# Soft and top-1 mixture of experts behind an attention stage: waits moved in the expert loop, one transpose a tile, a table with long runs, a sort with unit strides

## What is computed

```python
# attention, for each of 8 batches and 8 heads (S=512, Ns=32, D=64)
xread = softmax(x @ state.T / 8) @ state ; sread = softmax(state @ x.T / 8) @ x
x = concat(xread, sread)                        # 4352 rows of 512
# soft mixture: 32 slots, 4 for each of 8 experts
logits = x @ phi ; d = softmax(logits, over rows) ; c = softmax(logits, over slots)
slot_out[e] = relu((d.T @ x)[e] @ w1[e]) @ w2[e]
x = c @ slot_out
# top-1 mixture: each row goes to one of 8 experts
e = argmax(x @ w_gate) ; gate = softmax(x @ w_gate)[e] * sigmoid(x @ w_output_gate)[e]
out = gate * (relu(x @ v1[e]) @ v2[e])
```

## Time and profile before

| | |
|---|---|
| median of 3 runs | 518.16 us (517.82 to 519.98) |
| the profiled execution | 520.96 us, span 519.2 us |
| PE busy | 454.6 us, 88% of the span |
| PEld | 241.8 us |
| DVE, ACT, POOL | 132.7, 127.7, 127.8 us |
| the chain that ended last | PE 66%, DMA 14%, ACT 5%, issue 5%, DVE 5% |
| in it | output matmuls (858) 48%, the table's transfer 5%, weight units 5% |
| DMA | 87.20 MB, 168 GB/s over the span |

### The profile page before, as it was taken

How to read it: one execution, slowest core, us unless ns; L and a number is a source line. 1 busy time by engine, 2 the same in 40 slices (tenths; PEclk the granted TensorE clock), 3 DMA queues, 4 the chain that set the end, 5 groups by cost and what they waited for, 6 DMA issues and landing times.

```text
span 519.2 us, 9941 instructions
## 1 busy us (share of the span) xinstructions
PE 454.6 (88%) x3705; PEld 241.8 (47%) x3706; DVE 132.7 (26%) x315; ACT 127.7 (25%) x329; POOL 127.8 (25%) x191
## 2 busy tenths in 40 slices
PE   7888786799898793999999999999999999999991
PEld 5676655663435462444444444444444444444440
DVE  2689698820004601101010101010101010101000
ACT  3978554300001101212121212121212121212110
POOL 2433513040021004032222222232323232323110
PEclk9999898789796966999999999999999999999997
DMA  8799546779999998678601010101010101010110
GB/s 284 251 348 296 212 164 203 286 281 391 432 425 428 427 394 283 232 231 294 232 22 43 22 43 22 43 22 43 22 43 21 43 22 42 26 39 24 38 44 3
DMA packets 29306, 87.20 MB, mean 168 GB/s; under 512 B 5942, under 2 KB 15704, under 8 KB 26200
## 3 DMA queue, kind: packets, MB, share of 16 engines
q1 hardware_dynamic: 24016, 76.65, 39.3%
q0 software_dynamic: 3952, 9.49, 5.4%
q10 hardware_dynamic: 1304, 0.57, 0.4%
HBM read 77.25 MB, written 9.75 MB: 168 GB/s over the span
## 4 chain that ended last, share of the span: by engine, by line
PE 66%; DMA 14%; ACT 5%; issue 5%; DVE 5%; SPq 2%; POOL 1%; ACTq 0%; POOLq 0%; DVEq 0%
PE bank L858 48%; DMA token_rows<-z 5%; DMA arena<-in_moe_w 5%; DMA arena<-in_x 3%; PE bank L846 3%; PE bank L741 2%; SPq L287 2%; ACT z L1015 2%; PE bank L529 1%; PE bank L835 1%; DMA z<-token_rows,sidx 1%; PE bank L789 1%; PE bank L518 1%; PE bank L570 1%; PE bank L592 1%
## 5 line engine op out<-in xcount | busy, mean ns | idle before, releaser
L858 PE MATMUL bank<-arena,z 128*128 x560 | 249.3, 598 | 15.6 <-ACT z L1015 10.1
L858 PEld LDWEIGHTS bank<-arena,z 128*128 128x128 f32 x560 | 103.6, 190 | 139.6 <-issue 139.6
L1313 DVE TENSOR_SCALAR z<-bank 128x256 f32<-128x256 f32 x70 | 26.4, 419 | 260.2 <-PE bank L846 260.2
L1022 ACT ACTIVATE z<-bank,tile_gate 128x512 f32<-128x512 f32 x35 | 24.0, 687 | 242.0 <-PE bank L858 242.0
L449 POOL COPY rows_to<-sidx 128x1 int32 (+1 forms) x35 | 6.3, 181 | 167.9 <-ACT z L1022 167.9
L468 POOL DMA_INDIRECT out<-z,rows_to x35 | 36.7, 1049 | 29.8 <-POOL rows_to L449 29.8
L453 POOL DMA_INDIRECT z<-token_rows,rows_from x32 | 33.6, 1050 | 25.6 <-POOL rows_from L449 25.6
L846 PE MATMUL bank<-cT,parts 32*128 32x128 f32 x560 | 26.0, 300 | 0.0
L1015 ACT ACTIVATE z<-bank 128x256 f32<-128x256 f32 x70 | 23.0, 381 | 3.1 <-PE bank L846 1.1
L835 PE MATMUL bank<-ident,z 128*32 128x128 f32 x280 | 15.4, 292 | 9.1 <-DMA z<-token_rows,sidx 9.1
L846 PEld LDWEIGHTS bank<-cT,parts 32*128 32x128 f32 x560 | 19.2, 189 | 7.7 <-issue 7.7
(11 more groups left out here) (205 smaller groups left out, 416.5 us busy)
## 6 DMA issues: line engine op xcount, KB each, us to landing
arena<-in_moe_w SPq DMA_DIRECT2D x29, 2048.0 KB, 12.1
arena<-in_x SPq DMA_DIRECT2D x7, 1024.0 KB, 8.8
parts<-in_moe_w SPq DMA_DIRECT2D x3, 2048.0 KB, 13.1
arena<-in_x SPq DMA_DIRECT2D x2, 512.0 KB, 5.7
out<-z,rows_to POOLq DMA_INDIRECT x35, 3.0
token_rows<-z ACTq DMA_DIRECT2D x1, 528.0 KB
z<-in_state SPq DMA_DIRECT2D x1, 512.0 KB, 3.6
z<-in_state SPq DMA_DIRECT2D x8, 64.0 KB, 8.2
```

What stands on the lines that cost most here:

```text
L858: mm = e.matmul(pY[p][:, :], hT[p][:, c, :], arena[:, bass.ds(ex * UNIT + 512 * c, 512)], start=(c == 0), stop=(c == CF - 1))
L1022: e.activation(ysb[p], pY[p][:, :], ACT.Copy, scale=tile_gate[:, q:q + 1])\
L1313: e.tensor_scalar(hT[p][:, 2 * g:2 * g + 2, :], bank[g][:, 0:GW].rearrange("p (c t) -> p c t", c=2), 0.0, None, ALU.max).then_inc(relu_v, 1)
```

## The change

In the loop, TensorE's load of the expert's number and all waits for output(t) stand at the head of the step, ahead of turn_c(t+2) and hidden(t+1); the waits of hidden for the relu go, and each relu signals once instead of twice. The turning is one 128x128 transpose of `c4`, four copies side by side of the gathered rows, which VectorE lays out (`turned_rows`) behind its wait for the row. The table has a row of 34 floats: combine weights, gate, and the row's number in the output; it is written in one transfer with one contiguous run for each partition, and it begins with 102 rows that name no output row (`no_row`, written early through SP's queue). The sort gives the row's place in the table, as the upper bits of a float32; places that stay empty lead to such a row. The scatter takes its row numbers from the gathered rows. `lane_mat`, `tile_hot` and `tile_id` go: for each of 34 tiles VectorE writes `lane_hot[:, t, :]` and `tile_row[:, t, :]` with a scalar operation each, and TensorE's sort waits tile by tile. `count_experts` stands after expert 0 instead of 1. The foldings' operands are written chunk by chunk, so that they are read with unit stride. Three groups of `keep_clock` (4, 4, 6) stand in front of waits after w2. The first eight units (`EARLY = 8`) are loaded in four transfers each, of 4 KB a partition instead of 16 KB.

```diff
         def w_loaded(u):
-            return 16 * sum(1 for v in range(u + 1) if SLOT[v] == SLOT[u])
+            return 16 * sum(pieces(v) for v in range(u + 1) if SLOT[v] == SLOT[u])
...
-                e.dma_start(slot(SLOT[u]).rearrange("p (c n) -> p c n", c=c),
-                            src[ex].rearrange("(p c) n -> p c n", p=P)).then_inc(w_in[SLOT[u]], 16)
+                rows = src[ex].rearrange("(p c) n -> p (c n)", p=P)
+                step = UNIT // pieces(u)
+                for a in range(0, UNIT, step):
+                    e.dma_start(slot(SLOT[u])[:, a:a + step], rows[:, a:a + step]).then_inc(w_in[SLOT[u]], 16)
             for b in range(1, 4):
                 load_x(b)
+            e.wait_ge(no_row_ready, 2)
+            e.dma_start(table[0:FIRST_ROW, :], no_row[:, :]).then_inc(table_out, 16)
...
+            e.tensor_copy(rowbuf[:, :, GATE_W + 1], rowid[:, :]).then_inc(row_ready, 1)
...
-            e.wait_ge(w_used, 2 * NE)
-            e.tensor_copy(lane_mat, lane[:, :].unsqueeze(2).to_broadcast([P, P, NT])).then_inc(lanes_laid, 1)
...
-                numbers(rows_to[:, q % 2:q % 2 + 1], t, to_copied, t + 1)
+                e.tensor_copy(rows_to[:, q % 2:q % 2 + 1], gate_to[:, q, 1:2]).then_inc(to_copied, 1)
...
-                mm = e.matmul(pF[:, NS * c:NS * c + NS], every(siP, c, CD), foldn[:, :], start=True, stop=True)
+                mm = e.matmul(pF[:, NS * c:NS * c + NS], siP[:, P * c:P * c + P], foldn[:, :], start=True, stop=True)
...
             def sort_rows():
-                e.wait_ge(lane_ready, 3)
                 for t in range(NT):
-                    mm = e.matmul(pT[:, 0:2 * ST], lane_hot[:, :, t], tile_id[:, :, :, t], start=(t == 0),
-                                  stop=(t == NT - 1))
+                    e.wait_ge(lane_ready, 2 * t + 2)
+                    mm = e.matmul(pT[:, 0:ST], lane_hot[:, t, :], tile_row[:, t, :], start=(t == 0), stop=(t == NT - 1))
...
-                if ex == 1:
+                if ex == 0:
                     count_experts()
...
-                e.wait_ge(row_in[q], 4 * (t - q) + 16)
-                for g in range(4):
-                    mm = e.matmul(pC[NS * g:NS * g + NS, :], row[q][:, 0:NS], ident[:, :], start=True, stop=True)
-                mm.then_inc(c_psum, 1)
+                e.wait_ge(c4_ready, t + 1)
+                e.transpose(pC, c4[q % 2], ident[:, :]).then_inc(c_psum, 1)
...
-                if wait:
-                    e.wait_ge(relu_a, 2 * t)
-                    e.wait_ge(relu_v, 2 * t)
...
+            def output_free(t, ex, wait=True):
+                e.wait_ge(relu_a, t + 1)
+                e.wait_ge(relu_v, t + 1)
                 if wait:
                     e.wait_ge(y_copied, t - 1)
+                e.wait_ge(v2_ready, ex + 1)
...
             def step(t, q, first=False):
+                ex = expert(t)
+                output_free(t, ex, wait=not (first and q < 2))
                 with live_tile(e, live, t + 2):
...
-            for f in range(2):
-                e.dma_start(by_batch[4 * f:4 * f + 4, S:S + NS, :], rowbuf[:, NB * J + f, :]).then_inc(table_out, 16)
-            e.dma_start(by_batch[:, 0:S, :].rearrange("b (p j) w -> p b (j w)", j=J),
-                        rowbuf[:, 0:NB * J, :].rearrange("p (b j) w -> p b (j w)", b=NB)).then_inc(table_out, 16)
+            e.dma_start(table[FIRST_ROW:TABLE, :].rearrange("(p t) w -> p (t w)", p=P), z2[:, 0:NT * ROWW]).then_inc(table_out, 16)
...
+            for t in range(NT):
+                e.tensor_scalar(lane_hot[:, t, :], lane[:, :], dlane[:, t:t + 1], None, ALU.is_equal)\
+                 .then_inc(lane_ready, 1)
+                e.tensor_scalar(tile_row[:, t, :], lane[:, 0:ST], dtile[:, t:t + 1], code_f[:, t:t + 1], ALU.is_equal,
+                                ALU.mult).then_inc(lane_ready, 1)
...
+            def turned_rows(t, q):
+                e.wait_ge(row_in[q], 4 * (t - q) + 16)
+                if not isinstance(t, int) or t >= 2:
+                    e.wait_ge(c_psum, t - 1)
+                e.tensor_copy(c4[q % 2].rearrange("p (g n) -> p g n", g=4),
+                              row[q][:, 0:NS].unsqueeze(1).to_broadcast([P, 4, NS])).then_inc(c4_ready, 1)
```

More of the change, by code:

```diff
@@ L48 @@
 NU = 3 * NE
-LANES = SLOT[2 * NE - 1]
 def last_user(u):
@@ L432, in _ @@
             e.tensor_copy(rowbuf[:, :, 0:NS], comb).then_inc(row_ready, 1)
+            e.tensor_copy(rowbuf[:, :, GATE_W + 1], rowid[:, :]).then_inc(row_ready, 1)
             e.wait_ge(sit_psum, 1)
             e.memset(hTm, 0.0).then_inc(ht_zero, 1)
-            e.wait_ge(w_used, 2 * NE)
-            e.tensor_copy(lane_mat, lane[:, :].unsqueeze(2).to_broadcast([P, P, NT])).then_inc(lanes_laid, 1)
-            for q in range(4):
-                e.memset(row[q], 0.0).then_inc(row_zero, 1)
-            e.wait_ge(row_zero, 4)
-            e.wait_ge(sidx_ready, 1)
-            e.wait_ge(table_out, 16 * 3)
-            last_row = e.to_reg(ROWS - 1)
-            def numbers(to, t, copied, n):
-                e.sem_inc(turns, 1)
-                src = sidx[:, t:t + 1] if isinstance(t, int) else sidx[:, bass.ds(t, 1)]
-                e.tensor_copy(to, src).then_inc(copied, 1)
-                e.wait_ge(copied, n)
+            e.wait_ge(sidx_ready, 1)
+            e.wait_ge(table_out, 16 * 2)
+            last_row, last_out = e.to_reg(TABLE - 1), e.to_reg(ROWS - 1)
             def gather_row(q, rows):
@@ L457, in gather @@
                 e.wait_ge(gate_saved, t - 3)
-                numbers(rows_from[:, q:q + 1], t, from_copied, t - 3)
+                e.sem_inc(turns, 1)
+                src = sidx[:, t:t + 1] if isinstance(t, int) else sidx[:, bass.ds(t, 1)]
+                e.tensor_copy(rows_from[:, q:q + 1], src).then_inc(from_copied, 1)
+                e.wait_ge(from_copied, t - 3)
                 e.sem_inc(gathers, 1)
@@ L748, in _ @@
             for c in range(CF):
-                mm = e.matmul(pE[:, NS * c:NS * c + NS], every(hP, c, CF), fold[:, 0, :], start=True, stop=True)
+                mm = e.matmul(pE[:, NS * c:NS * c + NS], hP[:, P * c:P * c + P], fold[:, 0, :], start=True, stop=True)
             mm.then_inc(ht_psum, 1)
@@ L761, in _ @@
                 mm.then_inc(w_used, 1)
+            keep_clock(4)
             e.wait_ge(so_copied, 1)
             for c in range(CD):
-                mm = e.matmul(pT[:, P * c:P * c + P], every(soP, c, CD), fold[:, :, :], start=True, stop=True)
+                mm = e.matmul(pT[:, P * c:P * c + P], soP[:, P * c:P * c + P], fold[:, :, :], start=True, stop=True)
             mm.then_inc(sot_psum, 1)
+            keep_clock(4)
             e.wait_ge(sot_ready, 1)
@@ L772, in _ @@
             mm.then_inc(g2_psum, 1)
+            keep_clock(6)
             e.wait_ge(g2_ready, 4)
@@ L868, in step @@
                         hidden(t + 1, (q + 1) % 2)
-                output(t, q % 2, wait=not (first and q < 2))
+                output(ex, q % 2)
             turn_c(0, 0, wait=False)
             turn_c(1, 1)
-            hidden(0, 0, wait=False)
+            hidden(0, 0)
             keep_clock(10, pL)
```

130 lines of the change are left out of this document (63 added, 67 removed).

## The result

The changed kernel takes 488.43 us (median; 483.48 to 491.42) against 518.2 (517.82 to 519.98): ratio 0.9387, 95% interval 0.9311 to 0.9463. It is faster, by 29.8 us. The forecast was 484.7 in 479.5 to 496, so the time lies in the range and 3.7 us above the point. The profiled execution took 489.24 us, span 487.5.

What follows compares the result with a forecast made beforehand. Bounds: a front ending with the weights' stream, a loop start hanging on the table, 35 tiles bound by TensorE's sequence. Loop 23.0 plus start 10.5 saves 33.5: 520.96 to 487.5, median 2.8 lower, 484.7 us; range 479.5 to 496.

Steps and rivals of the forecast that it cites:

- (a): Loop, before output: load and waits moved ahead of the turning take the gap from +0.47 to -0.07, 0.54 us a tile.
- (b): Loop, turning: one transpose instead of 4 matmuls makes 0.35 us into 0.18, 0.17 saved a tile.
- R1: Rival, loop: the turning's 0.35 us is all exchange of tile forms; tile 8.07, kernel 490.1 us; chance 0.13.
- R3: Rival, loop: the gap before output isn't the sequencer's; tile 8.44, only 5.5 us saved there, 502.2; chance 0.05.
- (e): Start of the loop: the table in 128 runs of 4624 bytes takes 6.4 us instead of 27.85, there near 182.
- (f): Weights' stream before the loop: expert 7's unit lands at 190.3 us and its work ends at 192.7.
- (g): Sort: dlane ready at 173.0, 68 VectorE operations at 0.15 us each, sort ends near 186.5, sidx at 187.1.
- R4: Rival, sort: the 68 VectorE operations make the kernel slower from 0.74 us each, 522.6 us at 0.8; chance 0.03.
- (h): Gathered rows before the loop: first row at 191 us, third at 197.3.
- (i): TensorE from expert 7's end at 192.7 to the first output at 200.5 instead of 211.02: 10.5 us saved.
- R2: Rival, loop start: rows late or TensorE cold, first output at 205 to 206, kernel 489.7 us; chance 0.13.
- hidden or small: Front's other edits (foldings, keep_clock, small table DMA, 4 KB pieces): worth 0; pieces bounded by -1 and +1.5 us.

Runs made afterwards that it cites:

- b_waits: Kernel before with only the load of the expert's number and the waits for output moved ahead of the turning: 500.59 us, ratio 0.9662.
- a_short_runs: Changed kernel with the table written in nine transfers, 1152 runs of 544 bytes instead of 128 of 4624: 491.81 us, ratio 0.9531.
- a_slow_sort: Changed kernel with every lane_hot comparison made a second time, 34 more VectorE operations in the sort: 487.32 us, ratio 0.9431.
- a_v2swap: Changed kernel with v2 of expert 1 loaded ahead of expert 0's, the first tile waiting for that unit only: 480.65 us, ratio 0.9324.
- a_keep30: Changed kernel with 30 identity transposes instead of 10 ahead of the first tile: 487.36 us, ratio 0.9385.
- b_both: Kernel before with both loop edits, load and waits ahead of the turning and one transpose, nothing else: 493.73 us, ratio 0.9577.

## Why the prediction was right, and where it was off

**(a) waits ahead: right.** The gap went from +0.47 to -0.07, alone (b_waits) and in the whole change.

**(b) one transpose: right, with two small errors.** From turning to hidden it is 0.20 us, where 0.18 was forecast. The term beside it was mis-sized the other way: from output to turning it is 6.97, where 7.06 was taken over from before. b_waits, with the old turning, still has 7.06 (337.39 to 344.45), so this comes with the transpose; that it is the equal 128x128 form is the likely reason, not one that a run shows. Hidden to output is 0.66 as forecast. Together that is 7.83, the lower bound given, not 7.90. R1 (8.07) and R3 (8.44) are out.

**(c), (d): right.** In the loop's rows of the changed kernel TensorE waits for no copy and no row.

**The loop's sum** came out at 22.7 against 23.0, and that is luck: 33 intervals at 7.83 would have saved 2.5 more, and the half-clock first output (9.65 - 7.13) took them. Neither was in the sum.

**(e) the table: right in kind.** It was issued at 167.2, not 172, took 11 us (forecast: 10.3 with the term of up to 3.9; named as a sign: under 10), and is off the chain. The run length is the cause (a_short_runs): in short runs the table takes 26 us, near the bound of 27.85.

**(f) the weights' stream: right.** Expert 7's unit is there at 189.34 where 190.3 was forecast, and 1.05 us of that is the earlier front.

**(g) the sort: right to 3 us, by terms that were off.** dlane was ready at 168.9 (L1275 at 168.73, 0.20 long), not 173.0: expert 0's result was copied at 163.03, 4.1 us earlier than in before, which the sum took as unchanged. That gain, too, ends in the wait for the stream. One operation costs 0.18 us, not 0.15 (two in 0.37: L1280 at 169.03, next one at 169.40). The 34 sort matmuls took 0.03 each, not 0.07 to 0.15. The row that the 0.15 came from ran at a granted clock of 0.50, which the prediction didn't say; the new sort ran at 0.89. sidx came at 184.5 instead of 187.1. It decided nothing, as a_slow_sort shows: R4's price of 0.74 us an operation was a factor of four away, and at 0.18 the sort is not even on the path.

**(h), (i): the step that failed is the sentence behind them, "v2 of expert 0 lands 5 us behind expert 7's unit, at 195.5, and hides".** The landing was right (195.2). But the first tile isn't expert 0's. Which unit tile 0 needs follows from the input's routing, which the reference computes; it is the second, and that came 5 us behind the first, at 200.4. The sum before that sentence was good: with that wait taken away (a_v2swap), the front of before (102.92) and the distance of 96.8 make 199.7 us, where (i) said 200.5 with 1.1 for half clock. With the wait, 102.92 + 100.2 = 203.1, and the front started 1.05 us earlier: 202.03. R2 named the right place (a late, cold start, output near 205) for another reason; its sharper form, that identity transposes don't warm TensorE, doesn't fit the first output of a_keep30 (7.13), nor the changed kernel, whose ten transposes at 196.29 took 1.31 us, the full-clock time of (i).

**The front: "hidden or small" was half wrong.** The foldings were hidden as argued. They run twice as fast, and the time goes into waits for the same stream. These are rows of the changed kernel, two foldings and the last unit of w2:

```profile
110.45 1.05 PE L732 MATMUL bank<-foldn,z 128*128 128x32 f32 x8
...
127.93 1.97 PE L761 MATMUL bank<-fold,z 128*128 128x32 f32 x16 [0.81 <-DVE z L1198]
...
148.58 3.18 PE L771 MATMUL bank<-arena,z 128*32 128x512 f32 x16 [2.98 <-DMA arena<-in_moe_w]
```

Before had 2.05 and 4.01 us for the first two and 0.43 us of wait for the last unit of w2. The 4 KB pieces were given 0 with a bound of +1.5; they cost 3.2. The reason named for the bound, more issues on SyncE, is there (x(6) is issued 2.6 us later in the median), but x(5) was late before it. That the DMA engines move less for a full share with the pieces was not thought of. The other bound, a gain of 1 us through instruction fetches, showed in no run.

**Where the 3.7 us are.** 1.8 is the sum: 33.5 forecast, 31.7 found between the profiled executions (1.5 in the first output's start, 0.3 in the loop). The other 2.0 us is the step from the profiled execution to the median: before's profile was 2.8 us above its median, the changed kernel's only 0.8. The table shows what went with before's long profile: L678 at 102.92, where b_waits and b_both, with the same front, have 99.26 and 97.55. A late front goes through to the first output, as the nearly equal distances show. That the sum itself was off by only 1.8 is partly luck. At the start: the steps of (i) too late by 0.8, the front earlier by 1.05, the wait for v2 3.4 later, +1.6 together. In the loop: the first output 2.5 longer, the tile 33 x 0.07 = 2.3 shorter, +0.2.

**Open.** The fronts with whole units are 97.55 to 102.92 in the kernels with the rest of before's front, and 97.10 to 98.45 in the three with the changed one. Some of the other edits of the front may be worth 1 to 2 us, which the pieces then take back; no run separates this. That the pieces delay the inputs through what the DMA engines move is read from the windows; it was not tried apart, and it isn't traced how x(5) came to be issued 1.7 us later, nor why the changed kernel's delay grows from 2.2 us at the last input to 3.8 at L690 (medians of 98.11 and 101.87).

**A better kernel.** The changed kernel with EARLY = 0 is faster than both kernels and doesn't depend on the input's routing: 485.1 against 488.26 us on one chip, five of its six times below all six of the changed kernel (the two ratios to before, 0.9348 and 0.9396, have intervals that overlap, as before's own times spread from 516.11 to 522.65). a_v2swap's 480.65 shows what is still to be had where the first tile's unit of v2 comes in time.

## To carry to other kernels

An idle time ahead of a group of matmuls that comes after register work can be the sequencer's although the row names another engine: check the named releaser against the code's own wait, and put loads and waits a tile old ahead of work that must be issued anyway. Follow the data that the first unit of a loop needs, in this input, and not the first index of the loop. Take one fixed place upstream in several executions as the zero, and measure the edit by the distance from it; the draw of the front then cancels.

## What was not expected of the hardware

- Strided weights: a sort matmul with 82 columns and bf16 weights read at a stride of 34 cost 0.153 us at a granted clock of 0.50; at unit stride, with 41 columns, 0.032 (1.08 / 34) at 0.89. Stride, columns and clock changed together there. The fp32 foldings separate the stride: 16 in 1.97 us at unit stride, 4.01 strided. In before the clock fell from 1.00 to about 0.5 halfway through those 4.01 us, with TensorE busy throughout (1.00 from 131.5 to 133.5 us, 0.57 from 133.5 to 135.6), and both halves hold nine matmuls.
- Runs of 544 and 4624 bytes beside 16 KB transfers: 1152 of the first kept the last transfer in flight for 21.11 us, 128 of the second weren't waited for.
- Pieces of 4 KB on a queue that shares the engines with others: 313 to 331 GB/s for a full share from 36 to 66 us, where whole units had 335 to 343.
- Idle times of 2.86, 2.65 and 2.23 us behind identity transposes were followed by outputs of 9.65, 9.39 and 8.83 us, partly at the lower clock, and idle times of 4.49 and 4.40 by 8.61 and 8.66; one of 0.70 us was followed by 7.13.
